# The order of an attention unit's products on TensorE: scores' upper half first; outputs from state, upper half, lower half

## The reference, cut to what matters

```python
for t in range(S):                                     # attention, per batch and head
    state = alpha[:, :, t, :, None] * state + np.einsum('bhd,bhe->bhde', k[:, :, t], v[:, :, t])
    y[:, :, t] = np.einsum('bhd,bhde->bhe', q[:, :, t], state)
...
h = x @ w_in                                           # 384 -> 2048
x = (h * np.cos(h)) @ w_out                            # 2048 -> 384
...
h = np.maximum(np.maximum(x @ w1, x @ w2), x @ w3)     # 384 -> 768
out = h @ w_out                                        # 768 -> 384
```

## Time and profile before

| | |
|---|---|
| Time, median of 3 runs | 875.37 us (871.12 to 880.2) |
| The profiled execution | 873.21 us, span 871.6 us from its first to its last instruction |
| Mean granted TensorE clock | 0.990 |
| Busy: PE, PEld, DVE, ACT, POOL | 831.0, 757.8, 614.0, 421.7, 216.9 us |
| Attention units on TensorE | from 13.0 to 507 us |
| DMA | 54.35 MB, mean 62 GB/s |

### The profile page before, as it was taken

How to read it: one execution, slowest core, us unless ns; L and a number is a source line. 1 busy time by engine, 2 the same in 40 slices (tenths; PEclk the granted TensorE clock), 3 DMA queues, 4 the chain that set the end, 5 groups by cost and what they waited for, 6 DMA issues and landing times.

```text
span 871.6 us, 15664 instructions
## 1 busy us (share of the span) xinstructions
PE 831.0 (95%) x5446; PEld 757.8 (87%) x5446; DVE 614.0 (70%) x1286; ACT 421.7 (48%) x912; POOL 216.9 (25%) x242
## 2 busy tenths in 40 slices
PE   4688898999999999999999999999999999999998
PEld 3688798888888888888888878889999999999998
DVE  8698898777777777777776457757756566556454
ACT  3775555544454445444544456646343444434333
POOL 6564343333333332333233213310000000000000
PEclk9898999999999999999999999999999999999999
DMA  9633223202330132123213001130101010100001
GB/s 260 197 105 80 58 56 82 91 28 56 83 91 28 55 82 89 30 55 82 73 46 137 1 37 49 50 120 2 37 37 38 37 37 36 34 2 36 1 38 37
DMA packets 13780, 54.35 MB, mean 62 GB/s; under 512 B 1968, under 2 KB 2480, under 8 KB 13712
## 3 DMA queue, kind: packets, MB, share of 16 engines
q1 hardware_dynamic: 12992, 49.55, 19.5%
q0 software_dynamic: 720, 3.93, 1.1%
HBM read 44.04 MB, written 9.44 MB: 61 GB/s over the span
## 4 chain that ended last, share of the span: by engine, by line
PE 48%; DVE 1%; ACT 1%; issue 0%; POOL 0%; DVEq 0%; ACTq 0%
PE h_ps L1319 4%; PE score L1319 4%; PE h_ps L1321 4%; PE h_ps L1320 4%; PE score L1321 4%; PE score L1320 4%; PE h_ps L1226 2%; PE h_ps L1228 2%; PE h_ps L1227 2%; PE acc_pair L1226 2%; PE acc_pair L1228 2%; PE acc_pair L1227 2%; PE acc_pair L1301 1%; PE acc_pair L1300 1%; PE acc_pair L1299 1%; PE acc_last L1227 1%
## 5 line engine op out<-in xcount | busy, mean ns | idle before, releaser
L426 POOL TENSOR_TENSOR work<-work 128x512 f32<-128x512 f32 x75 | 96.1, 1281 | 259.6 <-DVE work L939 259.6
L573 ACT ACTIVATE work<-work 128x512 f32<-128x512 f32 (+1 forms) x112 | 63.6, 568 | 143.6 <-POOL work L426 114.1
L1226 PE MATMUL h_ps<-x_hi,w_hi 128*128 128x512 f32 (+1 forms) x312 | 121.6, 390 | 3.2 <-DVE x_lo L872 2.7
L925 DVE TENSOR_TENSOR work<-work,h_ps 128x512 f32<-128x512 f32 (+1 forms) x104 | 62.6, 602 | 76.0 <-ACT work L573 75.5
L1228 PE MATMUL h_ps<-x_lo,w_hi 128*128 128x512 f32 (+1 forms) x312 | 114.0, 365 | 0.0
L1227 PE MATMUL h_ps<-x_hi,w_lo 128*128 128x512 f32 (+1 forms) x312 | 113.5, 364 | 0.0
L1226 PE MATMUL acc_pair<-g_hi,w_hi 128*128 128x512 f32 (+1 forms) x224 | 83.6, 373 | 10.4 <-POOL g_lo L433 10.1
L806 DVE RECIPROCAL inv_decay<-decay 112x128 f32<-112x128 f32 x96 | 90.1, 941 | 0.1
L580 ACT ACTIVATE g_hi<-work 128x512 fp32r<-128x512 f32 (+1 forms) x112 | 63.4, 566 | 44.6 <-DVE work L925 39.4
L557 ACT ACTIVATE work<-h_ps 128x512 f32<-128x512 f32 (+1 forms) x104 | 54.7, 526 | 56.0 <-PE h_ps L1228 55.4
L1228 PE MATMUL acc_pair<-g_lo,w_hi 128*128 128x512 f32 (+1 forms) x224 | 81.6, 364 | 0.0
(11 more groups left out here) (205 smaller groups left out, 2390.3 us busy)
## 6 DMA issues: line engine op xcount, KB each, us to landing
v_all<-val SPq DMA_DIRECT2D x24, 576.0 KB, 4.1
raw<-qka SPq DMA_DIRECT2D x46, 288.0 KB, 5.1
block_out<-x SPq DMA_DIRECT2D x6, 768.0 KB, 3.3
x_in<-block_out SPq DMA_DIRECT2D x6, 768.0 KB, 4.4
raw<-wb SPq DMA_DIRECT2D x12, 384.0 KB, 3.0
out<-raw POOLq DMA_DIRECT2D x5, 768.0 KB, 3.5
stage_own<-wa SPq DMA_DIRECT2D x6, 384.0 KB, 6.6
x<-wa SPq DMA_DIRECT2D x6, 384.0 KB, 5.6
```

The lines of the kernel that those rows point to most:

```text
L426: nc.gpsimd.tensor_tensor(frac[:], turns[:], whole[:], ALU.subtract).then_inc(S["frac_done"], 1)
L573: nc.scalar.activation(cosine[:, cols], frac[:, cols], ACT.Sin, scale=-TURN if half else TURN).then_inc(S["cos_done"], 1)
L925: nc.vector.tensor_tensor(gated[:, cols], cosine[:, cols], h, ALU.mult).then_inc(S["g_done"], 1)
L1226: mm(ps, w_hi[:, w_at], xh, start=first, stop=False)
```

## The change

In `stage1` the two score products change places: the 64-column product of the upper keys is issued first, the 128-column product of the lower keys second, the transpose stays last. In `outputs` the first chunk's units keep their order. For all others the state product becomes the first (and clears the region), behind the wait for `mid_state`; then comes the wait for `mask_done`, the upper half, and the lower half as the last, which sets `y_done`. What is computed, the number of instructions, their shapes and the semaphores are the same.

```diff
                 if n >= FIRST_UNITS:
                     pe.wait_ge(S["state_done"], 2 * (n + 1 - inc_depth))
+                mm(ps[:, HIGH_AT], k_split[0:ROWS, p % 2, b, 1], q_dec[0:ROWS, p % 2, b, HALF:CHUNK], start=True, stop=True)
                 mm(ps[:, LOW_AT], k_split[0:ROWS, p % 2, b, 0], q_dec[0:ROWS, p % 2, b], start=True, stop=True)
-                mm(ps[:, HIGH_AT], k_split[0:ROWS, p % 2, b, 1], q_dec[0:ROWS, p % 2, b, HALF:CHUNK], start=True, stop=True)
                 nc.tensor.transpose(ps[:, KEYS_AT], k_dec[0:ROWS, p % 2, b],
                                     ident[0:ROWS]).then_inc(S["s_done"], 1)
...
-                pe.wait_ge(S["mask_done"], n + 1)
-                mm(y, v_all[:, p % 2, b, 1], scores[:, s, LOW_AT], start=True, stop=False)
-                last = mm(y[:, HALF:CHUNK], v_all[:, p % 2, b, 2], scores[:, s, HIGH_AT], start=False, stop=first)
-                if not first:
+                low = v_all[:, p % 2, b, 1], scores[:, s, LOW_AT]
+                high = v_all[:, p % 2, b, 2], scores[:, s, HIGH_AT]
+                if first:
+                    pe.wait_ge(S["mask_done"], n + 1)
+                    mm(y, *low, start=True, stop=False)
+                    last = mm(y[:, HALF:CHUNK], *high, start=False, stop=True)
+                else:
                     pe.wait_ge(S["mid_state"], n + 1 - UNITS)
-                    last = mm(y, state_mid[0:ROWS, s], q_dec[0:ROWS, p % 2, b], start=False, stop=True)
+                    mm(y, state_mid[0:ROWS, s], q_dec[0:ROWS, p % 2, b], start=True, stop=False)
+                    pe.wait_ge(S["mask_done"], n + 1)
+                    mm(y[:, HALF:CHUNK], *high, start=False, stop=False)
+                    last = mm(y, *low, start=False, stop=True)
                 last.then_inc(S["y_done"], 1)
```

## The result

The changed kernel is slower by 0.56%: the ratio of its times to those of the kernel before is 1.0056, with a 95% interval of 1.0033 to 1.0078. The medians of 22 runs each are 876.49 us (874.7 to 885.27) and 872.91 us (869.88 to 880.2). The forecast was 878.7 us with a range of 871.5 to 884, and +4.4 us; the ratio makes it +4.9 us (2.9 to 6.8), the medians +3.6. The profiled execution took 876.27 us (span 874.7), 3.1 more than that of before.

What follows compares the result with a forecast made beforehand. TensorE was taken to bound the four full steps. Full steps' scores 3.3, half step 0.8 and first units 0.3 gave +4.4 us: 877.6 on the profiled execution, 879.8 on the median, middle 878.7, range 871.5 to 884.

Steps and rivals of the forecast that it cites:

- TensorE bounds the full steps: From 165 to 508 us TensorE is busy for 341.7 of 343 us, so whatever its stream gains adds to the time.
- The transpose's load: Score products: the transpose's weight load runs beside the load ahead, so the second 64-column matmul hides it; 0.39 us, not 0.44.
- Scores' first part: Score products with the 64-column one first: 0.44 us against 0.39, +0.05 us a unit.
- Its product with 64 units: Scores' new order over units 32 to 95 of the four full steps: 64 x 0.051 = +3.3 us.
- Outputs, 0 by length: Output products, state product first, then upper, then lower: 0.61 us a unit, the same as before.
- The moved wait in the half step: Units 16 to 31, `mid_state` wait ahead of the outputs: between 0 and 1.7 us, taken as +0.8.
- part 1: The scores' upper half issued first, in all 96 units: +0.05 us a unit; 16 x 0.05 in the half step.
- The slow rival: Units 16 to 31: the moved `mid_state` wait feeds itself, 5.8 us, about +10 in all, 883 to 885; chance 0.09.
- The first 16 units: Units 0 to 15, only the scores' new order applies: between 0 and 1.0 us, taken as +0.3.
- The sum: Whole kernel: 3.3 + 0.8 + 0.3 = +4.4 us, written down as 878.7 us.
- The neutral rival: Score products: the transpose's load is an ordinary 0.11, a unit stays at 0.39; about 874 to 876 us; chance 0.28.
- the fast one: Score products: the short pair's loss belongs to the transpose alone; 0.33 a unit, -5.4 us, 868 to 870; chance 0.05.

## Why the prediction was right

**TensorE bounds the full steps: right.** The 0.05 us a unit came through there, and it is the largest part of the loss.

**The transpose's load (the step that the trace did not settle): right.** I read the loads at 301.84 and 301.89 as two that overlap. Three things bear it out: the load's listed time falls from 198 to 143 ns where nothing is ahead of it, a second transpose costs 0.10, and the kernels with the transpose moved alone are longer or nearly as short as the theory has it. What was never seen directly is the rule used for the sum, that a load has to be over before its own matmul runs; it rests on the distances, which it gives within 0.01 us in all five orders of the scores that were run. Had I gone by the rule that every load takes its columns over 1.2 GHz, as the Trainium skill has it ("TensorE: Matmul & The Clock Gate", "LDWEIGHTS (loading the stationary operand)"), the change would have been free. The rows agree with the rule for the ordinary loads (0.11 and 0.085) and disagree for the transpose's.

**Scores' first part, +0.051 us a unit: right**, 5.51 to 5.56. **Its product with 64 units, +3.3 us: 0.8 too much.** The full steps grew by 2.5, in every profile with the new scores. The term was taken for all 64 units. From increment to increment the twelve units in the middle of each step grow by 0.051 on average, but at the start of each step TensorE waits once for VectorE's state, and there the third unit follows 0.03 to 0.05 us sooner than before. The wait takes up a part of what is added ahead of it; it need not be all of the 0.8. TensorE's waits between 165 and 512 us, first before, then after:

```profile
PE score L1191 <- DVE state L837: 1.3, 4, 0.5
```

```profile
PE score L1191 <- DVE state L837: 1.0, 4, 0.4
```

**Outputs, 0 by length: right**, 0.61 us in both orders, and the changed kernel's full steps take as long as those with the new scores alone (349.5). With the old scores the new outputs take 0.4 us more there, for which I have no reason.

**The moved wait in the half step, 0 to 1.7 with part 1 in it and taken at 0.8: right, as far as the traces tell.** The wait for the scaled state did grow to 1.4 us (I had written about 1 us), in three places instead of six, and the half step is about 1 us longer in the traces. My statement before the last runs, that undoing the moved wait gives nothing back, was read from ratios too coarse for it; by the traces it gives back 0.5 to 1.8 us. That the price stays below the bound because VectorE's state is the later wait fits the waits of the two kernels, but no run shows it by itself. The slow rival, which wanted 5 us of this wait, is out.

**The first 16 units, +0.3: not seen**, 1.0002 with 2 us to each side, and nothing at unit 16 in the traces.

**The sum.** 4.4 us forecast, 4.9 by the ratio (2.9 to 6.8), 3.1 in the pair of profiled executions, of which the changed kernel's had the better clock. The traces account for about 3.5 us: 2.5 in the full steps and 1 in the half step. At equal clock the runs say 3.3 in the largest group and more in the smaller ones. So the sum is right in its mechanism and its main term; that it came out as near to the ratio as 0.5 us is luck, since one term was 0.8 too high and another shows nothing. The absolute forecast, 878.7, was 2.2 above the median of 22 runs for two reasons: its base, 874.3 between 873.2 and 875.4, lay 1.4 above the median of before, and its 4.4 is 0.8 above the 3.6 between the medians.

The neutral rival (0.39 a unit) and the fast one (0.33) are both excluded by the changed kernel's 0.44.

## What to carry to other kernels

Where short matmuls stand in a stream, look at each weight load and at the length of the matmul ahead of it: the load that is quickest belongs behind the shortest matmul, and the long loads behind long ones. A short matmul is best followed by a load that it can cover, and a wide matmul ahead of a quick load is cover thrown away. When a wait is moved forward, price it against the next wait on the same engine: if that one comes later, the moved one costs less than its own length.

## What the runs showed that I had not expected

A transpose's weight load of 128 columns goes through, by the estimate above, in some 0.06 us and starts beside the load ahead of it, while a normal fp32 load of the same tile shape takes 0.11; I had inferred it, but not that its listed time would show it so plainly (198, then 143 ns). In the kernel with two transposes four units between 16 and 29 us list 337 ns for this load behind a short pair and 224 ns behind a transpose; the granted clock at the last of them is 0.50.

```profile
L1195 PEld LDWEIGHTS h_ps<-ident,k_dec x4: 224/224/224, 16.2 to 28.5; 112*128 112x128 f32 x4
```

And a gap of 2.5 us in TensorE's stream at 86 us is enough, in some executions, for the clock to fall for the next stretch; the mean granted clock of a run explains much of its time, though at 0.992 the 34 runs of the kernel before still reach from 870.5 to 876.5 us. Where two kernels differ by 0.5%, it helps to compare runs of equal mean clock beside the medians.
